# An attention and adapter kernel whose whole instruction order and PSUM bank map are written out by hand, drawn up a second time

## The chip, the core and the metric

One core of a Trainium2 chip runs the kernel. The metric is device time in microseconds (us), the median of three runs. The core has TensorE (PE in the profile, with its weight loads as PEld), VectorE (DVE), ScalarE (ACT), GpSimd (POOL) and SyncE (SP). Each engine works through its own instructions strictly in order and waits on semaphores that other engines or transfers raise. PSUM, the only memory that TensorE writes, has eight banks of 128 x 512 fp32.

## The reference

Inputs q, k, v have shape (8 batch rows, 8 heads, 576 positions, 64). In heads 0 to 3 a position attends to itself and the 31 before it; in heads 4 to 7 it attends to every fourth position of the last 128. After that comes a mixture of low-rank adapters on the heads laid side by side (512 wide), with two experts of eight chosen for each token:

```python
scores = scale * np.matmul(q, k.transpose(0, 1, 3, 2))
scores = np.where(masks[None], scores, -1e9)          # masks by head, as above
attn = np.exp(scores - scores.max(-1, keepdims=True))
attn = attn / (attn.sum(-1, keepdims=True) + 1e-9)
x = heads_side_by_side(np.matmul(attn, v))            # 4608 tokens x 512
logits = x @ w_gate                                   # 8 experts
w = softmax over the two largest logits of a token
out = x + sum over those two e of w_e * (x @ A[e]) @ B[e]   # rank 16
```

## The kernel before

The eight batch rows go through the same chain, each in two groups of four heads (g = 0 plain, g = 1 dilated). An operation has a letter, then row and group: `S121` is part 1 of the scores of row 2, group 1.

- `L`, `Lk`, `Lq`, `Lw`, `Lv`: transfers of a row's q and k, or v, from HBM into one of four input buffers, issued by POOL (lines 273, 301, 305). They turn fp32 into bf16 on the way. A row that uses a buffer again waits for the scores and products of four rows before.
- `S0`, `S1` (PE): a mask product and the scores of five and of four blocks of 64 keys, 24 and 20 load-and-multiply pairs. `E0`, `E1` (ACT, line 351): exp from two PSUM banks into bf16.
- `V` (PE, 26 pairs): exp times v in three banks, the row sum in an extra column. `R`, `N` (DVE, lines 387 and 390): reciprocal and normalisation into the fp32 row buffer. `B` (POOL, line 397): bf16 copy.
- `T`, `U` (PE): transposes. `C`, `Cd`, `Cp` (ACT): copies of them to SBUF. `Z0`, `Z1` (PE): tokens times A and the gate weights. `Y` (ACT): copy out.
- `m`, `s12`, `tt`, `top` (DVE), `th` (ACT), `g2` (DVE), `gz` (POOL; DVE in row 7): the two best experts and the weighted rank-16 vector. `G` (PE) turns it, `gc` and `gn` (ACT) copy it, `D0`, `D1`, `D2` (PE) multiply it by B. `A` (DVE) adds that to the row buffer; in late rows `dy` and `dx` (ACT) copy parts of it and POOL adds them (`A53`, `A63`, `A73`: line 559).
- `O` (SP): the row goes out. `O0` to `O5` are whole rows of 1.15 MB, rows 6 and 7 go in two halves each. Every output waits for six of the eight transfers of row 7 (`late`), and an output of a whole row waits for the last but one before it.

At the start there are constants (`con`, `cc`, `cd`: masks; `awf`, `btf`: weights; `awc`, `btc`: bf16 copies), zeroed buffers (`pz`, `vz`, `xz`, `wz`) and scratch products on a zeroed buffer that nobody reads: `warm` (five) and `F0`, `F1`, `F2`, `F3` (two, two, one, one). A scratch product is fp32 and shows as two passes in the trace.

The order is a text, `PLAN`. Its words in sequence are the order of issue on each engine, and `@n` is the first PSUM bank of an operation; an operation waits until all users of its banks' former contents have finished:

```python
for b in range(o.bank.at, o.bank.at + o.bank.size):
    o.deps = o.deps + held[b]
    held[b] = list(o.bank.users)
```

Of the kernel before, what the change touches and what calls it, by code (L numbers as in the profile page):

```python
# [37 lines left out]
ASIDE = (4, 5, 6, 7)  # L38


FILL = (("S000", 2), ("V01", 2), ("S111", 1), ("S130", 1))

# [122 lines left out]
def program(nc=None, qkv=None, aw=None, bt=None, con=None, out=None):  # L167
# [4 lines left out]
    def sb(name, shape, dt):  # L172
        return nc.alloc_sbuf_tensor(name, shape, dt) if nc is not None else None
# [16 lines left out]
    G2 = [sb(f"g2{i}", [128, 5, 8], FP) for i in range(2)]  # L190
# [29 lines left out]
    def scratch(name, n, after, each):  # L220
        k = Bank(1)
        w = WARM[:, 0:256].bitcast(FP) if nc is not None else None
        add(name, "PE", ("x", each * n, 2 * n, "f", "f"), lambda: [
            mm(bank(k), w, w[:, 0:1].to_broadcast([128, 512]), True, True) for _ in range(n)][:0], after, k)

    scratch("warm", 5, ["wz"], 1.05)
    for i, (_, n) in enumerate(FILL):
        scratch(f"F{i}", n, ["warm"], 0.86)


# [369 lines left out]


PLAN = """
pz0 wz warm@4 F1@1 awf btf vz00 pz2 con vz10 Lk00 Lk01 Lv00 Lv01
S000@6 vz01 vz11 tab cc1 cd3 vz20 cc0 vz21 cd2 cd0 L11 pz1 E000
F2@1 L10 cd1 S100@4 S101@6 E100 E101 L2 Lw2 S001@2 E001 V00@4 R00 N00 V01@1
L3 Lw3 R01 F0@0 xz0 B00 N01 B01 T00@4 vz30 L4 Lw4 pz3 C00 S111@5 E111
awc S011@2 U0@0 T01@7 E011 V11@3 Cd0 Cp0 S010@1 C01 R11 vz31 E010 N11
Z00@0 Y00 m00 Z10@6 Y10 m10 S110@4 B11 s120 E110 tt0 th0 top0 V10@2
g20 gz0 T11@5 R10 N10 btc G0@1 gc0 D01@6 B10 gn0 D00@0 C11 xz1
U1@4 Cd1 Cp1 T10@5 C10 A01 A00 S121@6 E121 S120@3 S021@1 Z01@0 E021 Z11@5  # L610
Y01 m01 Y11 m11 L5 Lw5 s121 S020@1 D02@0 V21@5 E120 top1 tt1 th1 g21
E020 A02 V20@0 R21 N21 R20 gz1 G1@5 gn1 F3@6 S130@6 N20 gc1 B21 E130
S031@3 D12@2 E031 S030@0 D10@5 T21@7 E030 C21 A12 S131@3 B20 V30@0 A10 E131
U2@7 T20@6 R30 N30 Cp2 B30 L6 Lw6 V31@3 Cd2 C20 Z02@7 Y02 Z12@1 R31
N31 B31 T30@2 D11@6 Y12 C30 S041@4 A11 E041 S141@2 S140@6 m02 E141 S040@0
m12 s122 tt2 U3@5 Cp3 th2 E040 top2 Cd3 g22 gz2 V41@2 T31@0 E140
C31 V40@5 R41 N41 Z03@2 G2@0 Y03 gn2 Z13@1 gc2 R40 Y13 N40 B40
S051@2 D20@4 E051 A20 m13 S151@6 E151 Lq700 S050@0 S150@2 E150 m03 s123 V51@5
top3 tt3 T40@3 th3 Lq701 E050 C40 B41 g23 T41@4 C41 R51 Lq710 V50@0
N51 R50 D22@5 N50 U4@7 gz3 Cd4 Cp4 G3@6 gn3 D21@3 gc3 A22 A21  # L620
Z04@7 Y04 B50 Lq711 S060@0 D32@2 Z14@7 S161@5 m04 E060 Y14 m14 E161 s124
S160@0 A32 Lv710 T50@7 E160 D30@3 S061@5 top4 V60@0 A30 tt4 R60 C50 Lv711
O1 E061 B51 T51@3 N60 C51 V61@4 th4 g24 R61 N61 U5@7 S171@2 Cp5
Cd5 S070@0 Z05@7 E171 E070 Z15@6 Y05 S170@2 S071@4 Y15 Lv700 m05 m15 top5
Lv701 B60 gz4 E170 E071 s125 G4@0 B61 D31@6 tt5 th5 gn4 V70@1 T60@4
A31 gc4 V71@5 U6@0 C60 O0 g25 O2 gz5 G5@4 Cp6 Cd6 R70 N70
B70 T61@2 D41@0 D42@3 R71 N71 gn5 A41 C61 dx4 gc5 B71 Bx7 D40@5
Z06@2 Y06 Z16@4 Y16 A40 m06 A42 D52@3 m16 s126 dx5 top6 U7@7 Cp7
Cd7 tt6 T71@1 Cx7 C71 T70@4 D51@5 A52 th6 g26 A51 D50@0 A50 C70
gz6 Z07@2 Z17 m07 m17 s127 tt7 dy5 G6@5 gc6 O3 D61@0 th7 gn6  # L630
D62@7 A53 top7 O4 dx6 g27 D60@5 gy7 gz7 A62 dy6 O5 A61 A63
O61 G7@3 H7 gm7 gn7 gc7 D72@0 dx7 A72 D71@1 A60 D73@6 O60 A71
D70@7 O71 A70 dy7 A73 O70
"""

_INS = ["qkv", "aw", "bt", "con"]
# [64 lines left out]
```

## Time and profile before

| | |
|---|---|
| median of three runs (100.13, 100.55, 100.56) | 100.55 us |
| span of the profiled execution, first to last instruction | 99.2 us |
| runs above that span | 0.9 to 1.4 us |
| PE busy, load-and-multiply pairs | 81.6 us (82%), 1587 |
| ACT busy | 71.0 us (72%) |
| DVE busy | 62.3 us (63%) |
| POOL busy | 54.6 us (55%) |
| moved by transfers | 24.5 MB |

The profiled execution is one more execution than the three; what lies around its span shows only as the difference to the runs. A busy share is a mean over a stretch in which loads arrive, a middle in which PE is nearly always busy, and an end in which outputs leave.

### The profile page before, as it was taken

To read this page: it belongs to the slowest core of one execution; us is meant where nothing else is said; L and a number is where in the kernel's file an instruction comes from. 1 tells how busy PE (TensorE), PEld (TensorE's weight loads), DVE (VectorE), ACT (ScalarE), POOL (GpSimd) and SP (SyncE) were. 2 spreads that over 40 slices of the span, in tenths; PEclk is the share of its full clock that TensorE was granted. 3 is DMA by queue.
4 is the path that set the end of the run, shared out by engine and by line. 5 is a ranking of instruction groups with operands and counts; after the bars stand their busy time and mean duration, and the time that the engine had idled before them with its cause. 6 is when DMAs were issued, how large, how long until landed. Compare 5 with 4: busy or idle time off the path is not lost.

```text
span 99.2 us, 3611 instructions
## 1 busy us (share of the span) xinstructions
PE 81.6 (82%) x1587; PEld 59.9 (60%) x1587; DVE 62.3 (63%) x138; ACT 71.0 (72%) x123; POOL 54.6 (55%) x73
## 2 busy tenths in 40 slices
PE   3999969959569989999897979999799989766200
PEld 2443457548356765779676859878687878545100
DVE  5770007706468189359746697779676999979700
ACT  5195494399938983896997679989689899757200
POOL 5999900880549136404942297099085574637800
PEclk9999999999999999999999999999999999999975
DMA  2999999999999999999999999999979988979991
GB/s 33 300 204 208 207 214 226 201 217 220 211 211 211 214 219 213 219 216 206 210 217 212 224 212 214 210 204 175 198 264 412 415 353 360 426 297 401 420 422 76
DMA packets 5807, 24.50 MB, mean 247 GB/s; under 512 B 800, under 2 KB 928, under 8 KB 5024
## 3 DMA queue, kind: packets, MB, share of 16 engines
q0 software_dynamic: 3920, 14.23, 71.9%
q1 hardware_dynamic: 1728, 9.77, 23.9%
q10 hardware_dynamic: 144, 0.28, 1.0%
q8 instruction: 12, 0.20, 0.7%
q14 instruction: 3, 0.02, 0.1%
HBM read 29.07 MB, written 9.44 MB: 388 GB/s over the span
## 4 chain that ended last, share of the span: by engine, by line
PE 57%; ACT 18%; DVE 9%; DMA 5%; issue 3%; POOL 2%; POOLq 0%
PE ps L213 49%; ACT p L351 11%; PE ps L414 5%; DMA out_dram<-x 5%; DVE x L551 4%; DVE x L390 3%; ACT xt L424 2%; PE ps L504 1%; ACT zs L472 1%; POOL x L559 1%; ACT in L263 1%; POOL xb L397 1%; PE ps L438 1%; ACT xt L427 1%; DVE top L492 1%
## 5 line engine op out<-in xcount | busy, mean ns | idle before, releaser
L397 POOL CAST xb<-x 128x1152 bf16<-128x1152 f32 (+1 forms) x16 | 18.3, 1144 | 25.4 <-DVE x L390 25.4
L351 ACT ACTIVATE p<-ps 128x960 bf16<-128x960 f32 (+1 forms) x32 | 27.6, 899 | 4.2 <-PE ps L213 4.1
L213 PE MATMUL ps<-in,p 128*64 128x130 bf16 (+1 forms) x416 | 21.5, 221 | 3.7 <-ACT p L351 3.1
L390 DVE TENSOR_TENSOR x<-ps,rec 128x1152 f32<-128x1152 f32 x16 | 21.7, 1358 | 0.5
L213 PEld LDWEIGHTS ps<-in,p 128*64 128x64 bf16 (+1 forms) x416 | 17.1, 104 | 7.2 <-ACT p L351 4.1
L551 DVE TENSOR_TENSOR x<-x,ps 128x1024 f32<-128x1024 f32 (+1 forms) x16 | 17.5, 1116 | 3.4 <-PE ps L213 3.4
L387 DVE RECIPROCAL rec<-ps 128x18 f32<-128x18 f32 x16 | 4.3, 270 | 17.5 <-PE ps L213 17.3
L213 PE MATMUL ps<-warm 128*128 128x512 f32 x22 | 13.1, 737 | 1.5 <-DVE warm L217 1.5
L499 POOL TENSOR_TENSOR gz<-zs,g 128x640 bf16<-128x640 f32 x7 | 8.9, 1275 | 9.4 <-DVE g L494 9.4
L213 PEld LDWEIGHTS ps<-in 64*64 64x64 bf16 x576 | 10.9, 106 | 2.9 <-issue 0.9
L213 PE MATMUL ps<-in 64*64 64x96 bf16 (+1 forms) x576 | 11.9, 201 | 0.7 <-issue 0.7
L273 POOL DMA_DIRECT2D in<-in_qkv_dram x22 | 11.8, 581 | 0.8 <-POOLq L684 0.8
L213 PE MATMUL ps<-aw,xt 128*128 128x136 bf16 x160 | 11.2, 223 | 0.1
L424 ACT COPY xt<-ps 128x1024 bf16<-128x1024 bf16 x8 | 8.1, 1011 | 3.4 <-PE ps L414 3.3
L213 PEld LDWEIGHTS ps<-aw,xt 128*128 128x128 bf16 x160 | 9.6, 98 | 0.9 <-ACT xt L424 0.4
L414 PE MATMUL ps<-one,xb 128*128 128x128 bf16 x128 | 9.6, 219 | 0.6 <-issue 0.5
L414 PEld LDWEIGHTS ps<-one,xb 128*128 128x128 bf16 x128 | 7.6, 97 | 2.0 <-POOL xb L397 0.7
L213 PEld LDWEIGHTS ps<-warm 128*128 128x128 f32 x22 | 4.8, 235 | 6.6 <-issue 5.0
L427 ACT COPY xt<-ps 128x1024 bf16<-128x1024 bf16 x7 | 7.2, 1033 | 1.5 <-PE ps L414 1.5
L213 PE MATMUL ps<-bt,gn 128*128 128x256 bf16 (+1 forms) x48 | 6.8, 263 | 1.6 <-ACT gn L523 0.8
L213 PE MATMUL ps<-bt,gc 128*128 128x256 bf16 (+1 forms) x48 | 6.6, 255 | 1.5 <-ACT gc L520 1.5
L472 ACT COPY zs<-ps 128x408 f32<-128x408 f32 (+1 forms) x14 | 5.9, 457 | 2.0 <-PE ps L213 2.0
(55 smaller groups left out, 101.8 us busy)
## 6 DMA issues: line engine op xcount, KB each, us to landing
out_dram<-x SPq DMA_DIRECT2D x6, 1152.0 KB, 6.1
in<-in_qkv_dram POOLq DMA_DIRECT2D x5, 1152.0 KB, 22.1
in<-in_qkv_dram POOLq DMA_DIRECT2D x10, 292.5 KB, 23.1
in<-in_qkv_dram POOLq DMA_DIRECT2D x10, 288.0 KB, 8.2
out_dram<-x SPq DMA_DIRECT2D x4, 576.0 KB, 3.8
in<-in_qkv_dram POOLq DMA_DIRECT2D x10, 146.2 KB, 8.1
in<-in_qkv_dram POOLq DMA_DIRECT2D x2, 434.2 KB, 13.7
awf<-in_aw_dram ACTq DMA_DIRECT2D x1, 272.0 KB, 3.8
```

Source lines behind the costliest of these rows:

```text
L213: return nc.tensor.matmul(o, lhsT=lhsT, rhs=rhs, start=start, stop=stop, skip_group_check=True)
L273: nc.gpsimd.dma_start(out=IN[r % SLOTS][half(a), at : at + n], in_=qkv[r, a, :, at - 2 * VB * a : at - 2 * VB * a + n],)
L351: return [nc.scalar.activation(p[:, :, :].rearrange("p h (s c) -> p h s c", c=PER)[:, :, b0 : b0 + nb, 0:SEG], PS[:, k.at : k.at + 2, 0 : ...
L387: rc = add(f"R{tag}", "DVE", ("el", 60), lambda: [nc.vector.reciprocal(rec[:, :].rearrange("p (b i) -> p b i", b=3), PS[:, k.at : k.at + 3 ...
L390: nm = add(f"N{tag}", "DVE", ("el", XG), lambda: [nc.vector.tensor_tensor(X[r][:, XG * g : XG * g + XG].rearrange("p (b i n) -> p b i n", ...
L397: add(f"B{tag}", "POOL", ("el", cut), lambda: [nc.gpsimd.tensor_copy(XB[r % 2][:, g, 0:cut], X[r][:, XG * g : XG * g + cut])], [nm] + free)
L414: nc.tensor.transpose(tp[j][:, 128 * u : 128 * u + 128], xb[:, g, 256 * u + 128 * j : 256 * u + 128 * j + 128], ident())
L424: return [nc.scalar.copy(xt[:, 0:2, 0:S].rearrange("p j (c i) -> p j c i", c=C)[:, :, :, 0:128], tp.rearrange("p j (i c) -> p j c i", c=C))]
L427: return [nc.scalar.copy(xt[:, 2:4, 0:512], tp)]
L472: zc.append(add(f"Y{st}{r}", "ACT", ("el", len(us) * ZW), lambda us=us, k=k: [nc.scalar.copy(zs[:, us[0] : us[-1] + 1].rearrange("p u n -> ...
L499: return [en.tensor_tensor(GZ[i][:, us[0] : us[0] + n, :].rearrange("p u (e r) -> p u e r", e=E), zv()[:, us[0] : us[0] + n, 0:ER].rearran ...
L551: return [nc.vector.tensor_tensor(v, v, PS[:, k.at : k.at + nk].rearrange("p b n -> p (b n)"), ALU.add)]
```

## The change

The order text is replaced. The operations stay the same but for the scratch products: `F3` is gone, and the sizes are now 2, 1, 1 for `F0`, `F1`, `F2`. In front of the first scores stand only the five products of `warm`; `F1` (one) follows `S100`, `F0` (two) stays between `V01` and `T00`, `F2` (one) goes in front of `T01`, and nothing is left in front of `S130`, where `F3` was. Each engine's own order is new, and so are most bank numbers.

```diff
@@ -38,7 +38,7 @@
 ASIDE = (4, 5, 6, 7)
 
 
-FILL = (("S000", 2), ("V01", 2), ("S111", 1), ("S130", 1))
+FILL = (2, 1, 1)
 
 
 
@@ -224,7 +224,7 @@
             mm(bank(k), w, w[:, 0:1].to_broadcast([128, 512]), True, True) for _ in range(n)][:0], after, k)
 
     scratch("warm", 5, ["wz"], 1.05)
-    for i, (_, n) in enumerate(FILL):
+    for i, n in enumerate(FILL):
         scratch(f"F{i}", n, ["warm"], 0.86)
 
 
@@ -600,37 +600,35 @@
 
 
 PLAN = """
-pz0 wz warm@4 F1@1 awf btf vz00 pz2 con vz10 Lk00 Lk01 Lv00 Lv01
-S000@6 vz01 vz11 tab cc1 cd3 vz20 cc0 vz21 cd2 cd0 L11 pz1 E000
-F2@1 L10 cd1 S100@4 S101@6 E100 E101 L2 Lw2 S001@2 E001 V00@4 R00 N00 V01@1
-L3 Lw3 R01 F0@0 xz0 B00 N01 B01 T00@4 vz30 L4 Lw4 pz3 C00 S111@5 E111
-awc S011@2 U0@0 T01@7 E011 V11@3 Cd0 Cp0 S010@1 C01 R11 vz31 E010 N11
-Z00@0 Y00 m00 Z10@6 Y10 m10 S110@4 B11 s120 E110 tt0 th0 top0 V10@2
-g20 gz0 T11@5 R10 N10 btc G0@1 gc0 D01@6 B10 gn0 D00@0 C11 xz1
-U1@4 Cd1 Cp1 T10@5 C10 A01 A00 S121@6 E121 S120@3 S021@1 Z01@0 E021 Z11@5
-Y01 m01 Y11 m11 L5 Lw5 s121 S020@1 D02@0 V21@5 E120 top1 tt1 th1 g21
-E020 A02 V20@0 R21 N21 R20 gz1 G1@5 gn1 F3@6 S130@6 N20 gc1 B21 E130
-S031@3 D12@2 E031 S030@0 D10@5 T21@7 E030 C21 A12 S131@3 B20 V30@0 A10 E131
-U2@7 T20@6 R30 N30 Cp2 B30 L6 Lw6 V31@3 Cd2 C20 Z02@7 Y02 Z12@1 R31
-N31 B31 T30@2 D11@6 Y12 C30 S041@4 A11 E041 S141@2 S140@6 m02 E141 S040@0
-m12 s122 tt2 U3@5 Cp3 th2 E040 top2 Cd3 g22 gz2 V41@2 T31@0 E140
-C31 V40@5 R41 N41 Z03@2 G2@0 Y03 gn2 Z13@1 gc2 R40 Y13 N40 B40
-S051@2 D20@4 E051 A20 m13 S151@6 E151 Lq700 S050@0 S150@2 E150 m03 s123 V51@5
-top3 tt3 T40@3 th3 Lq701 E050 C40 B41 g23 T41@4 C41 R51 Lq710 V50@0
-N51 R50 D22@5 N50 U4@7 gz3 Cd4 Cp4 G3@6 gn3 D21@3 gc3 A22 A21
-Z04@7 Y04 B50 Lq711 S060@0 D32@2 Z14@7 S161@5 m04 E060 Y14 m14 E161 s124
-S160@0 A32 Lv710 T50@7 E160 D30@3 S061@5 top4 V60@0 A30 tt4 R60 C50 Lv711
-O1 E061 B51 T51@3 N60 C51 V61@4 th4 g24 R61 N61 U5@7 S171@2 Cp5
-Cd5 S070@0 Z05@7 E171 E070 Z15@6 Y05 S170@2 S071@4 Y15 Lv700 m05 m15 top5
-Lv701 B60 gz4 E170 E071 s125 G4@0 B61 D31@6 tt5 th5 gn4 V70@1 T60@4
-A31 gc4 V71@5 U6@0 C60 O0 g25 O2 gz5 G5@4 Cp6 Cd6 R70 N70
-B70 T61@2 D41@0 D42@3 R71 N71 gn5 A41 C61 dx4 gc5 B71 Bx7 D40@5
-Z06@2 Y06 Z16@4 Y16 A40 m06 A42 D52@3 m16 s126 dx5 top6 U7@7 Cp7
-Cd7 tt6 T71@1 Cx7 C71 T70@4 D51@5 A52 th6 g26 A51 D50@0 A50 C70
-gz6 Z07@2 Z17 m07 m17 s127 tt7 dy5 G6@5 gc6 O3 D61@0 th7 gn6
-D62@7 A53 top7 O4 dx6 g27 D60@5 gy7 gz7 A62 dy6 O5 A61 A63
-O61 G7@3 H7 gm7 gn7 gc7 D72@0 dx7 A72 D71@1 A60 D73@6 O60 A71
-D70@7 O71 A70 dy7 A73 O70
+con Lk00 Lk01 Lv00 Lv01 wz tab L11 awf L10 pz3 awc cc1 warm@6 vz31 cd1
+S000@0 vz20 L2 pz0 cd2 vz01 xz0 E000 S100@3 cc0 E100 F1@6 Lw2 vz10 cd0
+cd3 S101@3 pz1 xz1 E101 S001@5 vz00 V00@0 E001 R00 N00 B00 btf vz30
+V01@5 pz2 L3 R01 N01 B01 F0@3 T00@0 C00 S111@2 Lw3 S011@4 E011 E111 L4
+F2@1 T01@7 C01 Lw4 U0@6 Cp0 Cd0 vz11 V11@0 R11 N11 Z10@6 Y10 m10 btc
+Z00@7 Y00 S110@4 m00 s120 E110 B11 tt0 S010@0 top0 L5 E010 th0 g20 T11@3
+V10@4 R10 N10 vz21 gz0 C11 G0@0 gc0 B10 gn0 S121@1 E121 D02@6 A02 D00@3
+A00 U1@2 T10@0 Cp1 Cd1 C10 S021@5 D01@1 Lw5 E021 Z01@0 A01 Y01 Z11@7 Y11
+S020@1 m11 m01 top1 s121 tt1 th1 g21 gz1 E020 S120@3 E120 V21@5 S030@0
+E030 V20@2 R21 L6 N21 G1@5 gn1 S130@0 E130 B21 R20 N20 Lw6 D10@6 A10
+S031@1 gc1 E031 S131@3 D12@0 E131 A12 B20 U2@7 Cd2 T20@5 C20 Cp2 V30@0
+T21@3 C21 R30 N30 B30 V31@4 Lq711 Z12@7 R31 N31 B31 Y12 m12 Lq710 S141@0
+E141 D11@2 A11 T30@7 C30 Z02@6 Y02 m02 S041@4 E041 s122 tt2 th2 top2 g22
+S040@0 E040 Lq701 S140@6 E140 V41@2 T31@1 R41 N41 U3@0 Cp3 Cd3 V40@5 R40
+N40 gz2 G2@0 C31 Z03@1 Lv710 Lq700 gn2 B41 gc2 Y03 Z13@4 Y13 m03 m13
+top3 s123 B40 S151@2 S051@0 D20@5 E151 Lv711 E051 A20 O1 S050@2 E050
+T41@7 S150@0 V51@4 Lv700 U4@3 tt3 th3 C41 g23 gz3 R51 N51 E150 T40@7 C40
+V50@0 R50 N50 G3@7 Cd4 Cp4 Z14@6 gc3 Y14 Lv701 Z04@3 m14 gn3 Y04 m04
+S060@5 E060 D22@2 A22 B51 T51@1 C51 D21@3 A21 B50 U5@0 S161@6 O0 Cp5 Cd5
+top4 E161 s124 T50@5 S160@1 D30@3 C50 D32@0 E160 A32 S061@6 E061 Z15@5
+A30 tt4 th4 V60@0 R60 Y15 S171@6 N60 V61@3 R61 m15 N61 E171 S071@6 E071
+O2 Z05@2 Y05 g24 m05 B60 S070@0 B61 s125 tt5 gz4 S170@4 E070 D31@6 E170
+A31 th5 T61@3 C61 V70@0 U6@7 R70 Cp6 Cd6 top5 T60@3 g25 G4@4 N70 V71@5
+R71 C60 N71 Z06@3 gc4 gn4 Y06 Z16@1 Y16 m06 m16 s126 D42@0 top6 dx4 tt6
+D41@2 A41 Bx7 O3 gz5 G5@6 gc5 B70 T70@4 U7@5 th6 D40@0 Cp7 gn5 Cd7 g26
+C70 A42 A40 O4 B71 D50@2 dy5 A50 T71@6 Cx7 D51@0 A51 gz6 G6@4 A53 C71
+D52@2 gn6 dx5 A52 Z07@5 m07 Z17 m17 D60@2 O5 gc6 D62@1 dy6 s127 tt7 th7
+top7 g27 gz7 dx6 gy7 G7@0 H7 gn7 A63 gm7 A62 A60 O60 D61@6 D73@2 gc7
+D71@4 A61 O61 D72@1 A71 D70@0 dx7 A72 dy7 A70 A73 O71 O70
 """
 
 _INS = ["qkv", "aw", "bt", "con"]
```

## Rows read from the trace of the kernel before

**Rows 1.** Page: GB/s that the transfers moved, in 40 slices of 2.48 us.

```profile
GB/s 33 300 204 208 207 214 226 201 217 220 211 211 211 214 219 213 219 216 206 210 217 212 224 212 214 210 204 175 198 264 412 415 353 360 426 297 401 420 422 76
```

**Rows 2.** Page: DMA queue of instructions; packets, MB, share of 16 engines' span.

```profile
q8 instruction: 12, 0.20, 0.7%
```

**Rows 3.** Busy time by stretch: PE, PEld, DVE, ACT, POOL; PEclk, DMA share, GB/s.

```profile
23.00:45.00 22.00, 19.06 (x446) 14.62 (x445) 13.86 (x33) 17.82 (x30) 9.04 (x10) 1.00 1.06 215
45.00:70.20 25.20, 23.06 (x552) 18.56 (x547) 18.69 (x43) 21.01 (x34) 15.24 (x19) 1.00 1.04 208
```

**Rows 4.** Timeline of PEld, first 13 us: start, duration, instruction, [idle before].

```profile
1.49 0.50 PEld L213 LDWEIGHTS ps<-warm 128*128 128x128 f32 x2 [1.49 <-DVE warm L217]
...
6.78 0.21 PEld L213 LDWEIGHTS ps<-warm 128*128 128x128 f32 x1 [0.52 <-issue]
7.22 0.19 PEld L213 LDWEIGHTS ps<-warm 128*128 128x128 f32 x1 [0.24 <-issue]
...
10.33 0.11 PEld L213 LDWEIGHTS ps<-one 64*64 64x64 bf16 x4 [0.76 <-issue]
```

**Rows 5.** DMA issues begun at 1.92 and at 7.01: KB, us to landing.

```profile
in<-in_qkv_dram POOLq DMA_DIRECT2D x1, 288.0 KB, 6.0
...
in<-in_qkv_dram POOLq DMA_DIRECT2D x1, 146.2 KB, 11.4
```

**Rows 6.** Timeline of PE, 16 to 40 us.

```profile
16.59 1.94 PE L213 MATMUL ps<-warm 128*128 128x512 f32 x4
...
18.99 0.36 PE L213 MATMUL ps<-con,one 64*64 64x384 bf16 x4
...
26.56 1.33 PE L213 MATMUL ps<-in,p 128*64 128x130 bf16 x26 [1.21 <-ACT p L351]
...
38.61 1.08 PE L213 MATMUL ps<-warm 128*128 128x512 f32 x2
```

**Rows 7.** Timeline of ACT, 22.9 to 25 us.

```profile
22.96 1.16 ACT L263 COPY in<-warm 64x1170 f32<-64x1170 f32 x1
24.15 0.97 ACT L351 ACTIVATE p<-ps 128x960 bf16<-128x960 f32 x1
```

**Rows 8.** Timeline of PEld, 47 to 71 us.

```profile
47.15 0.45 PEld L414 LDWEIGHTS ps<-one,xb 128*128 128x128 bf16 x8
...
52.78 0.37 PEld L414 LDWEIGHTS ps<-one,xb 128*128 128x128 bf16 x6 [0.63 <-issue]
...
58.74 0.11 PEld L213 LDWEIGHTS ps<-in 64*64 64x64 bf16 x3 [0.87 <-issue]
...
70.18 0.15 PEld L213 LDWEIGHTS ps<-in,p 128*128 128x128 bf16 x2 [0.67 <-issue]
```

**Rows 9.** DMA queue of instructions in the window 50.3 to 51.4 us.

```profile
q8 instruction: 1, 0.02, 5.4%
```

**Rows 10.** Timeline of all engines, 75.8 to 99.2 us.

```profile
77.98 1.34 PE L213 MATMUL ps<-in,p 128*64 128x130 bf16 x26
...
85.97 1.36 PE L213 MATMUL ps<-aw,xt 128*128 128x136 bf16 x20
...
86.56 1.27 POOL L559 TENSOR_TENSOR x<-x,in 128x512 f32<-128x512 f32 x1
...
88.18 0.24 ACT L491 ACTIVATE th<-tt 128x40 f32<-128x40 f32 x1
...
92.98 1.26 POOL L559 TENSOR_TENSOR x<-x,btf 128x512 f32<-128x512 f32 x1 [0.24 <-DMA out_dram<-x]
```

**Rows 11.** DMA issues running at 88.0 and at 94.4: KB, us to landing.

```profile
out_dram<-x SPq DMA_DIRECT2D x1, 1152.0 KB, 5.0
...
out_dram<-x SPq DMA_DIRECT2D x1, 576.0 KB, 4.1
```

**Rows 12.** Busy time by stretch (columns as in rows 3), end of loads, outputs.

```profile
71.50:73.50 2.00, 1.98 (x63) 1.61 (x60) 1.97 (x4) 1.58 (x5) 1.22 (x2) 1.00 0.60 153
...
90.00:97.50 7.50, 1.68 (x20) 1.09 (x17) 3.48 (x5) 2.09 (x5) 3.81 (x4) 0.87 0.96 395
```

## The prediction

> **What bounds the kernel now.** I read the page first. The bandwidth by slice shows two regimes [rows 1]: loads at about 213 GB/s from 5 us to 72 us without a hole, then outputs at about 400. So the transfers are busy all the time, and a gain in the arithmetic can only come out where an engine is late behind them. Next the table by stretch [rows 3]. From 23 to 45 us PE is busy 19.06 of 22.00 us and ACT 17.82; from 45 to 70.2 PE is busy 23.06 of 25.20. Up to 23 us the chain runs after landings; from 23 to 45 PE and ACT pass waits to each other; from 45 on PE alone sets the pace until the last exp-times-v product, V71, which ends at 79.32 (77.98 + 1.34) [rows 10]. After it comes a chain of some 15 us through DVE, ACT, PE and POOL to the last output.
>
> The third view is PE's own idle time. Three holes in the busy stretch have no releaser, only "issue": before 52.78, 58.74 and 70.18 [rows 8]. Each lies inside one operation (six of T31's eight transposes, three of S050's 24 pairs and two of V60's 26 are still to come), so no semaphore explains it. Counting pairs in the old order, they are at pairs 856, 982 and 1236: 126 and twice 127 apart. The instruction queue moved 12 packets in all [rows 2], 1587 pairs over 12 packets are 132 a packet, and one packet moved between 50.3 and 51.4, shortly before the first hole [rows 9]. I read these holes as PE out of instructions until the next packet is in. Pair 728 was at 47.2 (two transposes into T30) [rows 8], so the stretches between packet edges took 5.6 us (728 to 856), 6.0 (856 to 982) and 11.4 (982 to 1236). If a packet cannot be turned around in less than about 5.7 us, PE's pace in the dense stretch is set by that and by no order.
>
> **The change part by part.** All sums are differences to the profiled span of 99.2 us; they are then taken from the median of 100.55, which lies 1.3 above it.
>
> *Front.* Two products, four passes of 0.43 us (6.78 to 7.22) [rows 4], go. Of the ten left, six start at the slow pace before 6.78 and four run after it, so S000 can begin at 6.78 + 4 x 0.435 = 8.5 in place of 10.33. Its own q and k land at 1.92 + 6.0 = 7.9 [rows 5], so the landing allows it: -1.8 us. That gain meets the next landing. The last piece of L11 lands at 7.01 + 11.4 = 18.4 [rows 5]; S111 began at 18.99, queued behind F0 (1.94 us) and T00 [rows 6]. In the new order F0 starts some 1.6 us earlier and T00 is over by 17.5, so S111 starts at the landing: -0.6, the whole of what the front can hand on. What else moved there is hidden: awf goes behind the table load, so awc, now in front of pz0, vz01, vz10, pz1 and vz00 on DVE, ends near 6.8, and these end near 11, before V00 at about 12.3. Should awf be 1.3 us later still, V00 slips with it, and the 0.6 stays untouched until T00 is 0.9 late.
>
> *Rows 0 to 3.* A zeroing copy of 1.16 us on ACT (vz31) stood in front of E010 [rows 7]; it moves into the idle front, and vz21 comes in behind th0, where ACT would wait for T11 and gz0 anyway: 0. F2, about 1.0 us now in front of T01, is covered by the exps that V11 waits for; without that cover it would cost up to 1.0. Walking the new order with durations of the trace: S111 18.4, S011 to 19.4, E011 (0.97) [rows 7] and E111 to 21.2, V11 (1.33) to 22.55, Z10 and Z00 (1.36) to 23.95, S110 and S010 to 24.9, E110 and E010 to 26.2. So V10 begins at 26.25 where it began at 26.56 [rows 6]: -0.3. Half the gain has gone, because Z now stands in front of the scores and E010 is the last exp instead of E110. On the way to V20 the new order puts more in front of it (D01, S120, S030, and th1 ahead of E020, so E020 waits for the chain m, s12, tt): V20 is about 0.3 late. Then F3 is missing (1.08 us) [rows 6], and V30 and V31 come out 0.6 to 0.7 early. In front of V31 both orders hold the same set of operations but for the scratch products. After V31 the new order brings only Z12 and 18 pairs of S141 to pair 728: 46.2 to 46.5 in place of 47.2. I take -0.85; the bounds are -1.0 (no wait for a packet) and 0 (the 0.3 waits before V10 and V20 doubled).
>
> *Rows 4 to 7.* Without packet holes the same walk brings pair 1236 (in V60) at 68.2, -2.0. With the packet interval the gain stays what it was at pair 728, because the old order was at the packets' pace from 728 to 1236 (23.0 us for 508 pairs) and the new one needs the same packets: -0.85. The Trainium skill bears on this, "Runtime: NRT & Kernel Launch", section "Instruction fetch mechanics": blocks of 16 KiB are fetched while the block before runs, and crossing an edge is "mostly hidden". By that rule the sum at pair 1236 would be -2.0; the trace disagrees in three places with 0.5 to 0.7 us of PE idle each [rows 8]. I go by the rows. From pair 1236 to the end of V71 the new order has 221 pairs, the old 207 (T61 and U6 now stand ahead of V70 and V71): +0.45 at some 31 pairs a microsecond. V71 ends at -0.4.
>
> *The end.* Counted from V71's end, the old order had Z07 at 6.65, th7 at 8.86, A53 over at 8.51 and A73 over at 14.92 [rows 10]. Walked with the same durations the new one has Z07 at 6.5, th7 at 8.95 (behind gc6 and dy6 on ACT), A53 over at 7.2 with A52 at 8.2, A73 over at 15.05. The last outputs keep the transfers full, 0.96 from 90 to 97.5 [rows 12]; O5, which starts that train and took 5.0 us to land [rows 11], leaves 0.3 earlier, the last one leaves 0.1 later and took 4.1. I take -0.25, bounds -0.5 and +1.2 (below).
>
> *Loads and outputs.* POOL issues row 7's loads behind V31 and not between casts near the end. Slices 26 to 28 ran at 204, 175 and 198 GB/s [rows 1]; against 213 that is (9 + 38 + 15) / 213 x 2.48 = 0.7 us, which the first output may win. It does not reach the end, since O5 waits for A53: 0, bound -0.7. The pause between loads and outputs (share 0.60 in 71.5 to 73.5) [rows 12] stays, as the same six transfers hold back O1.
>
> Sum: -0.85 + 0.45 - 0.25 = -0.65, so 100.55 - 0.65 = 99.9.
>
> **The rivals.** *The packets don't bind.* If the holes were put there by something else, or fall where PE waits anyway, the -2.0 at pair 1236 stands, with +0.45 - 0.25 a total of -1.8; transfers left unused 0.8 us at 71.5 to 73.5 [rows 12], and the earlier loads give 0.7, so they allow about 1.5 to 1.8: 98.8. Against it: three holes, evenly spaced in pairs. It is what the section of the Trainium skill named above ("Runtime: NRT & Kernel Launch", "Instruction fetch mechanics") leads one to expect. *Nothing arrives.* The 0.6 from L11's landing is used up by V20 (the walk has it 0.3 late there already), F3's 1.08 us only lay where PE waited for exps, and the packets keep the old pace: 0, 100.5. For it: ACT is at 81% from 23 to 45 [rows 3], and every exp has a copy in front. *Slower: ACT in the tail.* The new ACT order puts dy5 before C71, and gn6, dx5, gc6, dy6 before th7. If gn5, which D50 and so dy5 wait for, ends more than about 0.4 us later than in my walk, C71 and Z07 slip by 0.85 and th7 waits for dy6 another 0.5; G7, H7 and all that follow on the last chain move 1.2 to 1.4 us. Less the 0.4 at V71 that gives 101.3. For it: five more copies stand in one engine's queue ahead of a step that everything left waits for. Against: in the walk D50 is over 0.3 to 0.4 us before ACT gets to dy5, a small margin, but it is there.
>
> **How the numbers follow.** Likeliest 0.46 at 99.9, its own range 99.4 to 100.4. Packets not binding 0.16 at 98.8. Nothing 0.20 at 100.5. Slower 0.18 at 101.3. A half per cent, 0.5 us, is about what can be told from no change: faster means under 100.05, slower over 101.05. Of the likeliest, two thirds lie below 100.05: 0.30; with 0.16 that is 0.46, rounded 0.47. The rest of the likeliest, 0.16, and most of nothing, 0.17, give 0.32; slower 0.18 and the upper edge of nothing, 0.03, give 0.21. The range 98.7 to 101.3 holds the likeliest, nothing, most of the first rival and half of the slower one.
>
> **What would show it.** S000 at 8.2 to 8.6; S111 at 18.3 to 18.5, whatever came before; V10 near 26.2, V20 near 37.2, V31 near 44.0; PE idle with "issue" alone inside U3 or V40, T41 and V60 (pairs 856, 982, 1236), at 51.5 to 52.5, 57.5 to 58.5 and 69 to 70; V71 over near 78.9; th7 near 88; the last output issued near 94. If the holes sit at other pairs or are gone, the packet step is wrong and the time is below 99.4. If V31 is not before 44.4, the middle gave nothing. If th7 is more than 9.5 us behind V71's end, the tail has become the bound. A PE clock below 1.00 in the stretches before 90 us, where every row shown has 1.00 [rows 3, 12], would mean that the missing products were needed after all: then every PE term here is wrong, and upwards.

## The result and the profile after

| | before | after |
|---|---|---|
| median of the runs | 100.56 us (4 runs) | 104.40 us (103.61 to 104.83, 4 runs) |
| ratio, 95% interval | | 1.038 (1.032 to 1.044) |
| span of the profiled execution | 99.2 us | 102.7 us |
| V71 over | 79.32 | 81.82 |
| last output leaves, lands | 94.32, 98.43 | 98.96, 101.87 |

The kernel is 3.8% slower; 99.9 was forecast, with 101.3 as the upper end. Times here and below are medians of all runs; disturbed executions are left out of every ratio, and the traces of e2, e3, c3 and q2 show such ones. In the two traces the loss has two places: 2.50 us at V71's end and another 0.94 from there to the last landing, 3.44 together.

The page first: GB/s by slice, the granted clock by slice, the instruction queue.

```profile
PEclk9999999999999999999999999999999999998555
GB/s 44 273 208 206 210 221 205 215 213 215 212 216 210 218 212 213 216 212 216 218 208 216 215 213 215 210 208 183 196 438 416 409 384 32 280 401 269 397 296 201
q8 instruction: 12, 0.20, 0.7%
```

Loads run at the same 213 GB/s to the same time [rows 1]; the output phase has a new gap (32 GB/s in slice 33). Busy time by stretch, columns as in [rows 3]:

```profile
23.00:45.00 22.00, 18.58 (x448) 14.42 (x446) 14.40 (x33) 18.48 (x30) 10.64 (x12) 1.00 1.06 215
45.00:70.20 25.20, 22.02 (x516) 17.83 (x520) 16.09 (x41) 20.09 (x36) 13.39 (x16) 1.00 1.05 213
...
86.00:88.00 2.00, 1.49 (x16) 1.26 (x17) 2.00 (x4) 2.00 (x5) 1.54 (x2) 1.00 0.00 0
...
94.00:96.00 2.00, 1.64 (x11) 0.75 (x8) 1.50 (x2) 0.54 (x2) 0.00 (x0) 0.56 0.65 270
```

Up to 45 us as many pairs are done as before; from 45 to 70.2 PE does 516 in place of 552 and is busy a microsecond less. The clock is 1.00 until 94 us, when it falls to the lower level. From the timeline of PEld, where S000 begins:

```profile
7.94 0.11 PEld L213 LDWEIGHTS ps<-one 64*64 64x64 bf16 x4 [0.90 <-DMA in<-in_qkv_dram]
```

From the timeline of PE, S111, V10 and the end of V71 (80.48 + 1.34 = 81.82):

```profile
18.62 0.36 PE L213 MATMUL ps<-con,one 64*64 64x384 bf16 x4 [1.38 <-DMA in<-in_qkv_dram]
...
26.32 0.77 PE L213 MATMUL ps<-in,p 128*64 128x130 bf16 x18
...
80.48 1.34 PE L213 MATMUL ps<-in,p 128*64 128x130 bf16 x26
```

S000 begins 2.4 us earlier [rows 4], at the landing of its q and k; S111 waits for its landing and begins 0.37 earlier, V10 0.24 [rows 6]. Next the holes, from the timeline of PEld, 45 to 73 us:

```profile
45.99 0.36 PEld L213 LDWEIGHTS ps<-in 64*64 64x64 bf16 x15
46.92 0.10 PEld L213 LDWEIGHTS ps<-in 64*64 64x64 bf16 x1 [0.57 <-issue]
...
53.18 0.10 PEld L414 LDWEIGHTS ps<-one,xb 128*128 128x128 bf16 x1 [1.10 <-issue]
...
59.41 0.37 PEld L414 LDWEIGHTS ps<-one,xb 128*128 128x128 bf16 x6 [0.93 <-issue]
...
66.07 0.19 PEld L213 LDWEIGHTS ps<-in 64*64 64x64 bf16 x12 [0.75 <-issue]
...
71.86 0.87 PEld L213 LDWEIGHTS ps<-in,p 128*64 128x64 bf16 x17 [0.36 <-issue]
```

Where the old kernel has three holes without a releaser [rows 8], this one has five, in S141, T31, T41, S060 and V60. Counted in pairs they are at 729, 855, 983, 1108 and 1235. Measured between the starts of neighbouring weight loads beyond the usual 0.05, they are 0.63, 1.15, 0.97, 0.80 and 0.42, in sum 3.97 us (before: 0.68, 0.93 and 0.72, 2.33).

The chain of waits, from V71's end to the last output (start, duration, what):

```profile
84.07 0.50 DVE top L492
84.57 0.55 DVE tt L489
85.13 1.13 DVE x L551
86.26 0.11 DVE g L494
86.37 1.14 DVE x L551
87.51 0.05 issue
87.56 0.61 PE ps L213 x4
...
90.92 0.25 ACT th L491
91.17 0.02 issue
91.20 1.24 DVE g L494
...
93.07 0.75 PE ps L504 x10
...
94.60 1.86 PE ps L213 x9
...
97.62 1.26 POOL x L559
```

A41 and A40 (L551) now stand behind row 6's selection (`top6`, `tt6`) on DVE, so A40 is over at 87.5 and O4 leaves at 87.53 (before 83.92); hence the two microseconds at 0 GB/s. `g27`, 0.20 us before, takes 1.23. The timeline of all engines shows what runs beside it, and how long four products took at the lower clock, 1.06 us in place of 0.60 to 0.61 elsewhere:

```profile
91.11 1.26 POOL L559 TENSOR_TENSOR x<-x,in 128x512 f32<-128x512 f32 x1 [0.90 <-ACT in L557]
91.20 1.23 DVE L494 SCALAR_TENSOR_TENSOR g<-th,top 128x40 f32<-128x40 f32 x1 [0.33 <-ACT th L491]
...
95.00 1.06 PE L213 MATMUL ps<-bt,gc 128*128 128x256 bf16 x4
```

### The profile page after: what moved, and what is told of

It is laid out like the page before. It is cut to its first block, busy times and chain, and to the rows that moved or that the text cites. A ratio compares the mean times of both kernels' runs of the same rounds, so it can differ in the third digit from the quotient of the medians.

```text
span 102.7 us, 3601 instructions
## 1 busy us (share of the span) xinstructions
PE 81.2 (79%) x1583; PEld 59.7 (58%) x1583; DVE 63.1 (61%) x138; ACT 71.2 (69%) x123; POOL 54.0 (53%) x73
## 4 chain that ended last, share of the span: by engine, by line
PE 35%; DMA 28%; DVE 11%; ACT 11%; POOL 5%; issue 5%; POOLq 0%
PE ps L213 29%; DMA in<-in_qkv_dram 28%; ACT p L351 6%; DVE x L390 4%; PE ps L414 3%; POOL in L273 3%; DVE x L551 2%; PE ps L504 2%; ACT xt L424 2%; DVE g L494 1%; POOL x L559 1%; POOL xb L397 1%; ACT xt L427 1%; DVE rec L387 1%; ACT zs L472 1%
## 5 line engine op out<-in xcount | busy, mean ns | idle before, releaser
L397 POOL CAST xb<-x 128x1152 bf16<-128x1152 f32 (+1 forms) x16 | 17.8, 1114 | 27.1 <-DVE x L390 27.0
L551 DVE TENSOR_TENSOR x<-x,ps 128x1024 f32<-128x1024 f32 (+1 forms) x16 | 17.7, 1116 | 2.3 <-PE ps L213 2.1
L414 PE MATMUL ps<-one,xb 128*128 128x128 bf16 x128 | 10.1, 219 | 2.5 <-issue 1.7
L213 PE MATMUL ps<-warm 128*128 128x512 f32 x18 | 10.9, 741 | 1.2 <-DVE warm L217 1.2
L213 PE MATMUL ps<-bt,gn 128*128 128x256 bf16 (+1 forms) x48 | 7.3, 278 | 2.8 <-ACT gn L523 1.5
L213 PE MATMUL ps<-con,one 64*64 64x384 bf16 (+1 forms) x64 | 6.0, 362 | 2.8 <-DMA in<-in_qkv_dram 1.4
L523 ACT COPY gn<-ps 128x576 bf16<-128x576 bf16 (+2 forms) x9 | 5.2, 593 | 3.4 <-PE ps L504 3.4
L472 ACT COPY zs<-ps 128x272 f32<-128x272 f32 (+1 forms) x14 | 6.2, 455 | 1.7 <-PE ps L213 1.6
```

The costliest lines, as they stand in the source:

```text
L213: return nc.tensor.matmul(o, lhsT=lhsT, rhs=rhs, start=start, stop=stop, skip_group_check=True)
L397: add(f"B{tag}", "POOL", ("el", cut), lambda: [nc.gpsimd.tensor_copy(XB[r % 2][:, g, 0:cut], X[r][:, XG * g : XG * g + cut])], [nm] + free)
L414: nc.tensor.transpose(tp[j][:, 128 * u : 128 * u + 128], xb[:, g, 256 * u + 128 * j : 256 * u + 128 * j + 128], ident())
L472: zc.append(add(f"Y{st}{r}", "ACT", ("el", len(us) * ZW), lambda us=us, k=k: [nc.scalar.copy(zs[:, us[0] : us[-1] + 1].rearrange("p u n -> ...
L551: return [nc.vector.tensor_tensor(v, v, PS[:, k.at : k.at + nk].rearrange("p b n -> p (b n)"), ALU.add)]
```

## The experiments

Theory A (A1 beside A2 below) from these rows: PE cannot get its next packet of instructions sooner than some 6 us after the last one while loads run, whatever the order; an order that reaches the edge of a packet early is starved there, and again at each edge after it. Rivals: row 7's loads, now queued earlier on POOL, slow the packets or the loads (A2); the missing scratch products cost something; the new end alone makes the loss.

**Row 7's loads put back late, and the same loads put early in the old order.**

```diff
 e1_late7 (new order)
-... V31@4 Lq711 ... m12 Lq710 ... E040 Lq701 ... Lv710 Lq700 ... Lv711 ... Lv700 ... Lv701
+... B40 Lq711 Lq710 ... gz3 Lq701 ... B50 Lv710 Lq700 Lv711 Lv700 Lv701
 e2_early7 (old order)
+... gz2 Lq711 Lq710 Lq701 Lv710 Lq700 Lv711 ... B40 Lv700 Lv701
```

> The new order with one thing put back: POOL issues row 7's eight transfers behind B40, gz3 and B50 (about 58 to 69 us) in place of behind B30 to gz3 (46.7 to 61.8); PE, ACT and DVE orders stay as in the new kernel. Theory A2 (the instruction packets take longer because row 7's loads are queued so early): the holes without a releaser at T31, T41, S060 and V60 shrink from 1.1, 1.0, 0.8 and 0.5 us to the 0.5 to 0.7 of the kernel before, V71 ends at 80.0 to 80.5 in place of 81.8, and the time is 102.6 to 103.0. Theory A1 (the packets are slow beside any loads, whenever these were issued): holes unchanged within 0.2 us, V71 at 81.5 to 82.0, time 104.1 to 104.7.

> The cross test: the old order, with row 7's eight transfers issued early, behind gz2 and B40 (about 52.7 to 58.5 us in place of 57.4 to 69.3). A2: the holes in S050, S060 and V60 grow by 0.3 to 0.5 us each, V71 ends about 1.0 to 1.5 later than 79.3 and the time is 101.5 to 102. A1: V71 stays at 79.3 within 0.3; the loads are in up to 0.7 us earlier, and the time is 100.2 to 100.7.

Measured: e1 103.91 us, ratio to before 1.026 (1.014 to 1.037, overlapping with the changed kernel's), holes of 1.52, 1.14, 0.98 and 0.79 at the first four edges, V71 over at 82.31. e2 100.92, ratio 1.003 (0.997 to 1.008). The place of these loads is not the cause; A2 falls. A1 holds at three of the four holes; the first grew by 0.9, and V71 and the time lie 0.3 and 0.2 outside its ranges. e1's trace shows one thing more: from 67 to 69 us, where its transfers are busy only 0.60 to 0.67 of the time, the packet after the edge at 67.01 starts 1.7 us behind that edge, in place of 3.8 to 4.3 behind the three before it, and the next edge has no hole.

**No loads beside the middle.** Loads of rows 4 to 7 left out in both orders; the outputs wait for S171.

```diff
     def loads(r):
+        if r >= SLOTS:
+            for g in range(2):
+                qk_ready[r, g], v_ready[r, g] = [], []
+            return
...
+    late.append("S171")
```

> The new order without the loads of rows 4 to 7: these rows compute on the data that rows 0 to 3 left in the buffers, and the outputs, which had waited for row 7's loads, wait for S171. Theory A (PE runs out of instructions because its packets queue behind loads): from about 40 us, when row 3 is in, to S171 no hole without a releaser is over 0.2 us; a packet follows its edge by under 2.5 us in place of 3.5 to 4.3; V71 ends 3.5 to 4.5 us earlier than 81.8. Theory B (the new order's own waits between PE, ACT and DVE set the pace): V71 at 81 or later, with the idle time moved to waits that have a releaser.

> The kernel before without the loads of rows 4 to 7 (they compute on what rows 0 to 3 left; outputs wait for S171), the partner of the run of the new order without them, in which V71 ended at 77.97. Theory A: no holes without a releaser; the old order loses its 1.8 to 2.3 us of holes less what other waits take up, so V71 at 77.4 to 78.4, at most 0.5 away from the new order's. Then without packets the two orders are alike and the packets make all of the 2.5. Theory D (the new middle is slower in itself): V71 at 76.5 or below.

Measured, one run each: new order 101.12, old order 100.06. Busy time from 45 to 68 us, the new order (e5):

```profile
45.00:68.00 23.00, 22.47 (x543) 18.52 (x544) 17.17 (x42) 21.17 (x37) 9.45 (x8) 1.00 0.01 3
```

The same for the old order (e9):

```profile
45.00:68.00 23.00, 22.09 (x536) 17.85 (x537) 16.85 (x43) 19.93 (x34) 9.31 (x8) 1.00 0.01 3
```

With the transfers idle (share 0.01) no hole of over 0.2 us without a releaser is left in either at the packets' edges, though the pairs and packets are the same. In e5 a packet starts 0.3 to 1.5 us behind its edge, in the changed kernel 3.5 to 4.3 while loads run. PE is past the edge near pair 1236 at 67.9 us in the new order, where the walk without packets had 68.2, and at 68.1 in the old: up to there the two orders are alike without loads, and the holes come of packets that have to get through beside loads. V71 is over at 77.97 in the new order and 77.22 in the old. These 0.75 us, more than the 0.5 that Theory A allowed, arise behind pair 1236, where the new order has T61 and U6 in front of V71. The Trainium skill ("Runtime: NRT & Kernel Launch", "Instruction fetch mechanics") has them "mostly hidden": true of these two runs, not of the kernels with loads.

**The edges moved.** 40 one-column scratch pairs behind F1 shift every later operation against the packets.

```diff
+    for h in range(2):
+        kp = Bank(1)
+        add(f"X{h}", "PE", ("x", 1, 20, "f", "f"), lambda h=h, kp=kp: [
+            mm(PS[half(i % 2), kp.at, i : i + 1], WARM[half(h), 0:64], WARM[half(h), 0:1], True, True) for i in range(20)][:0], ["wz"], kp)
...
-... E100 F1@6 ...
+... E100 F1@6 X0@7 X1@2 ...
```

> The new order with 40 scratch pairs of one column more, behind F1, where PE waits 1.2 us for S101 anyway. A (holes at the edges of instruction packets): they stay at the same pair counted from the start (about 729, 855, 983, 1108, 1235) and so move 40 pairs back in the order: out of S141, T31, T41, S060 and V60 into V31 or Z12, V41, D20 or S050, Z14 or Z04, and D30 to S061. If something about those operations makes the holes, they stay in S141, T31, T41, S060 and V60, at pairs 769, 895, 1023, 1148 and 1275. The time stays within 0.7 us of 104.4 in both.

Measured, one run: 105.92 us, above the 0.7 around 104.4 that was expected. Three of the holes, timeline of PEld:

```profile
50.69 0.14 PEld L213 LDWEIGHTS ps<-in 64*64 64x64 bf16 x6 [0.81 <-issue]
...
57.28 0.18 PEld L213 LDWEIGHTS ps<-in 64*64 64x64 bf16 x10 [0.90 <-issue]
...
63.34 0.10 PEld L213 LDWEIGHTS ps<-in,p 128*128 128x128 bf16 x1 [0.67 <-issue]
```

They stand at pairs 856, 983 and 1110, within two of the changed kernel's, but in S140, S051 and V50; a fourth (1.72) is at 1236, in S061. At 729 there is none here. The holes belong to the count of instructions and not to an operation or its banks.

**The orders spliced.** New up to V31 and then old (c1), new up to V71 and then old (c3), old up to T61 and then new (c2).

```diff
 c1_newfront: words of the new order to V31@4, then the old order's other words
 c3_new_oldtail: words of the new order to V71@5, then the old order's other words
 c2_old_newtail: words of the old order to T61@2, then the new order's other words
```

> The new order and banks up to V31, from there the old ones for all that is left (scratch products as in the new kernel). It has the front's gain (V31 ends 0.5 earlier than in the kernel before, 45.5 in place of 46.0) and the old middle and end. Theory A (from the edge at pair 728 on the packets of instructions set the pace, so an early arrival there is worth nothing): V71 ends at 79.0 to 79.8 against 79.3, time 100.2 to 100.9. Rival D (the new middle order itself costs the 2.5 us, and the front's gain is real): V71 at 78.6 to 78.9, time 99.8 to 100.1.

> The new order up to V71, the old one behind it (A41 and A40 ahead of m06 to tt6 and g2 of row 6; dy5 behind C70, th7 ahead of dy6; A53 and A63 where they were). If the new end costs 0.95 us by itself (19.1 us from V71's end to the last output's landing before, 20.05 after), V71 ends at 81.5 to 82.4 and the last landing follows by 18.9 to 19.3: time 103.2 to 103.8. If the end is as long whatever its order because the outputs bound it, it follows by 19.8 to 20.2: 104.1 to 104.8.

> The cross test: the old order up to T61, the new one behind it (G5 where the new one has it). If the new end costs 0.95 us by itself: V71 at 79.3, time 101.2 to 101.8. If it costs nothing in a kernel whose V71 is early: 100.3 to 100.8.

Measured: c1 101.59, ratio 1.008 (1.005 to 1.011); c3 103.05, 1.020 (1.013 to 1.027); c2 104.36, 1.035 (1.029 to 1.042). c1's holes (PEld):

```profile
47.56 0.10 PEld L414 LDWEIGHTS ps<-one,xb 128*128 128x128 bf16 x1 [0.26 <-issue]
...
53.52 0.15 PEld L414 LDWEIGHTS ps<-one,xb 128*128 128x128 bf16 x2 [1.09 <-issue]
...
60.02 0.11 PEld L213 LDWEIGHTS ps<-one 64*64 64x64 bf16 x3 [1.24 <-issue]
```

V31 is over at 45.66 there, 0.36 early, and V71 at 80.95, 1.6 late, with everything behind V31 in the old kernel's order: 1.0 late by pair 1236, the rest with a wait of 0.93 for a DVE normalisation before 75.63 that the old kernel has not. So the new front by itself turns its gain into a loss, a small one (0.8%). The new end taken off the new kernel gives back about 1.8%. c2's 3.5% is no price of the new end: its chain goes from V71 through T61, a copy and Z06 to row 6's selection, while the changed kernel has T61 ahead of V70; th7 begins 11.03 us behind V71's end (9.10 in the changed kernel), and the last landing follows by 21.97 (20.05). All three forecasts of the time missed, c3's by 0.15.

**The scratch products alone.** Taken out of the old order (p1), put back into the new one (p2).

```diff
 p1_old_noscratch (old order)
-pz0 wz warm@4 F1@1 awf ... S000@6
+pz0 wz warm@4 awf ... S000@6
 p2_new_scratch (new order)
-... warm@6 vz31 cd1 S000@0
+... warm@6 vz31 cd1 F3@1 S000@0        (F3: two products)
```

> The old order and old banks, with the two scratch products in front of S000 taken out and nothing else changed: the headline of the change alone. Theory A (PE is starved at every instruction packet once it reaches an edge early): S000 starts near 8.5 instead of 10.33, S111 at L11's landing (18.4 to 18.6), the middle is 0.3 to 0.6 us early at pair 728 (T30), a hole of 0.3 to 0.6 us appears there, and what follows is not earlier than in the old kernel or up to 0.8 us later, as in the kernel that had the new order up to V31 (0.8 % slower): 100.5 to 101.3 us. Rival B (what costs is the new order of operations, not the earlier arrival): the 0.4 to 0.6 us of the front stay and the kernel takes 100.0 to 100.2 us. A third possibility: the products were needed for the clock; then the clock in the records falls below 1.00 before 20 us.

> The new order with two scratch products put back in front of S000, nothing else changed. S000 starts near 9.7 instead of 7.95 and S111 is 0.3 to 1.0 us later. Theory A (packets set the pace, the time is fixed from the first starved edge on): V31 ends 0.3 to 0.8 us later than in the changed kernel, the hole in S141 is smaller by about as much, and from the hole in T31 on both run alike: V71 within 0.4 us of 81.8, the time 104.0 to 104.8. Rival B (the earlier front is itself what costs, because PE loses its lead at pair 728): without the hole in S141 the later edges come 0.5 us or more earlier each, V71 ends near 80.5 to 81.2 and the time is 103.0 to 103.7.

Measured: p1 100.67 beside 100.78, ratio 0.998 (0.995 to 1.002). p2 103.86, ratio 1.026 (1.020 to 1.033). PEld of p1 at its holes:

```profile
58.09 0.11 PEld L213 LDWEIGHTS ps<-one 64*64 64x64 bf16 x3 [0.71 <-issue]
...
70.01 0.39 PEld L414 LDWEIGHTS ps<-one,xb 128*128 128x128 bf16 x7 [0.94 <-issue]
```

V71 in p1's timeline of PE:

```profile
77.60 1.34 PE L213 MATMUL ps<-in,p 128*64 128x130 bf16 x26
```

PEld of p2 at the first edge:

```profile
47.70 0.13 PEld L213 LDWEIGHTS ps<-in 64*64 64x64 bf16 x5 [0.89 <-issue]
```

In p1 V31 is 0.5 us early, pair 728 is crossed at 46.9 without a hole, and V71 is 0.38 early [rows 10]: in this one trace the gain lasts, as the prediction had it, though over twelve runs it can't be told from none. The 0.5 at V31 is no larger than the scatter: other traces of the old front have it over at 45.54 (e2) to 46.38 (c2). The hole that Theory A put at 728 did not appear; neither did Rival B's time. In p2 the hole in S141 is larger (0.95), which neither expected, V71 is over at 82.01, which is Theory A's number, and the time lies between the two forecasts. Put back, the scratch products change the ratio from 1.038 to 1.026, with intervals that just touch; taken out of the old order they cost nothing. The order makes the loss.

**Inside the new end.** A62 in front of A63 on POOL (e3); A40's add cut to 64 columns (q2).

```diff
 e3_tail
-... gn7 A63 gm7 A62 A60 ...
+... gn7 gm7 A62 A63 A60 ...
 q2_a40cut
+                if (r, g) == (4, 0):
+                    return [nc.vector.tensor_tensor(v[:, 0:64], v[:, 0:64], PS[:, k.at, 0:64], ALU.add)]
```

> The new order with one exchange on POOL: A62 in front of A63. In the new kernel g2 of row 7 took 1.22 us in place of 0.20, beginning 0.09 us behind A63's start (91.11) and ending 0.05 us behind its end (92.37). Theory C (that DVE instruction, with two inputs in SBUF, is held while POOL works): A62 can't begin before dx6 ends (91.43), so g27 begins alone and takes 0.20 us; gz7, G7 and the rest move 1.0 us forward and the time is 103.2 to 103.6. Rival (POOL's A63, A62 and then O60 bound the end, or the outputs do): g27 is short but the end stays, 104.2 to 104.6.

> The new order with the add A40 cut from 1024 columns to 64 (so the output of row 4 is not complete in its other columns); it is the add that holds row 4's output and D51 back until 87.5 us in the changed kernel. Theory E (the chain A41, A40, D51, G6 behind row 6's selection on DVE sets the end): O4 leaves near 86.4 instead of 87.53, D51, G6 and the copies behind it come 0.6 to 1.1 us earlier, th7 and G7 too, and the time is 103.3 to 103.8. Rival (the end is set by Z07's branch and by g27, which stands beside A63 on GpSimd): O4 leaves 1.1 us earlier, but G7 and the last output move by 0.3 us or less, and the time is 104.0 to 104.6.

e3's `g27` and A63 (timeline of all engines):

```profile
91.78 0.20 DVE L494 SCALAR_TENSOR_TENSOR g<-th,top 128x40 f32<-128x40 f32 x1 [0.33 <-ACT th L491]
...
92.77 1.27 POOL L559 TENSOR_TENSOR x<-x,in 128x512 f32<-128x512 f32 x1
```

With POOL out of its way `g27` is back at 0.20. G7 follows V71's end by 10.2 us in place of 11.25, and the last output leaves at 97.75, 15.3 behind V71 in place of 17.1; but it takes 4.6 us to land, 19.94 behind V71 in all (20.05), and e3's times (103.47 to 105.10) scatter too widely to price it. So the hold is real; e8 below shows what it is worth in the total. In q2 O4 leaves 4.70 us behind V71's end in place of 5.71, while `g27` still takes 1.23 and G7 comes 11.03 behind V71 (11.25): the rival's reading. The time, 104.85 with a ratio of 1.029 (1.022 to 1.036), overlaps with the changed kernel's, so no gain is claimed for it. From these two traces only distances within each are used.

**Fewer pairs.** Masks by two 128 x 128 products in place of four 64 x 64, in the new order (e6), the old one (e7), and with A62 first (e8).

```diff
-                for pr, a, c in tiles:
-                    mm(PS[half(c), k.at + pr, 0 : nb * SEG], ident(a), mask(a), True, False)
+                for pr in range(2):
+                    mm(PS[:, k.at + pr, 0 : nb * SEG], ident(), mask(), True, False)
```

> The same edit in the new order. A: 32 pairs fewer ahead of the first starved edge (S141) and 24 fewer from there to V60: V71 ends 1.2 to 1.8 earlier than 81.8, time 102.5 to 103.2. B: V71 within 0.3 of 81.8, time 104.0 to 104.8.

> The old order with fewer PE instructions for the same work: each score operation adds its mask with two products of 128x128 (both halves of the partitions at once, the mask is the same in both) in place of four of 64x64, so it has 22 and 18 pairs in place of 24 and 20; 64 pairs of 1587 go, the columns that stream through PE in that time stay about the same (0.36 to 0.40 us an operation before). Theory A (in the dense stretch a block of some 127 pairs takes about 6.2 us, since the next packet of instructions is not there earlier): fewer pairs are worth time though PE works no less; the holes in T31, S050 and V60 shrink or go, V71 ends 0.8 to 1.2 earlier than 79.3, time 99.4 to 99.9. Theory B (the work of the array sets the pace): V71 within 0.3 of 79.3, time 100.3 to 100.9.

> The new order with the two-product masks and with A62 in front of A63 on POOL. If g27's 1.2 us beside A63 lie on the chain that ends last, this is 0.8 to 1.1 us below the run with the masks alone; if the outputs bound the end, it is the same within 0.4.

Measured: e6 106.33, ratio 1.052 (1.046 to 1.058); e7 107.63, 1.066 (1.061 to 1.072); e8 105.98, 1.049 (1.043 to 1.055). e6 and e7 are slower than their parents, and both forecasts missed. e8 lies 0.35 us below e6, within the 0.4 that was expected if the outputs bound the end: `g27` takes 0.20 in e8 and 1.23 in e6, G7 comes 1.0 earlier behind V71, and the last landing follows V71's end by 20.08 and 20.03. What slows e6 and e7 is in each score operation (e7, PEld):

```profile
40.79 0.23 PEld L213 LDWEIGHTS ps<-in 64*64 64x64 bf16 x16 [0.32 <-issue]
41.07 0.11 PEld L213 LDWEIGHTS ps<-con,one 128*128 128x128 bf16 x2
41.58 0.27 PEld L213 LDWEIGHTS ps<-in 64*64 64x64 bf16 x20 [0.40 <-issue]
```

At the change from products on the whole array to 64 x 64 tiles the next weight load stands 0.32 or 0.40 us, 32 times in the kernel, 11.4 us in sum; PE meanwhile finishes the mask products. That outweighs 64 pairs fewer, and says nothing on Theory A.

## Why the prediction was wrong

*Front*: the gain was there, by another path than forecast. S000 began at 7.94 and not at 8.2 to 8.6: the scratch passes reached the faster pace at 5.56 and not at 6.78, the last began at 6.86, and the landing of q and k ended the wait, not the products. S111 stood at L11's landing as forecast, 18.62 (18.3 to 18.5).

*Rows 0 to 3*: right in PE's arrival. V10 26.32 (26.2), V20 37.48 (37.2), V31 44.21 (44.0), and PE stood in front of pair 729 at 46.24, as forecast (46.2 to 46.5). It then waited until 46.92, where the old order crossed at 47.15: of the -0.85 only some -0.2 was left. These are single traces: V31 was over at 45.54 to 46.38 in four of the old front and at 45.54 to 46.52 in seven of the new, so the front's gain is no larger than that scatter.

*Rows 4 to 7* is the step that failed: "With the packet interval the gain stays what it was at pair 728". Two things were wrong in it. First, it counted the interval from pair 728, where the old order was not starved. The edge before, pair 601, is crossed at 41.0 us by both orders, counted in the two traces. The new order runs the 127 pairs after it in 5.3 us, the old one in 6.2. The packet started at 44.5 in both and would let PE go on at about 46.9, 5.9 us behind the edge. The gain at 728 was made inside one packet interval and could not be kept. Second, the interval was taken as 5.7. In the new trace PE goes on after the edges at 46.92, 53.18, 59.41, 66.07 and 71.86: 5.9, 6.3, 6.2, 6.7 and 5.8 us, a mean of 6.18 from 41.0, starved at each. The old order, starved at three of five, took 29.2 us over the same five, 5.84 each [rows 8]. Five times 0.34 is 1.7 us: PE is past the edge near pair 1236 at 71.86 and not 70.18, +1.7 where the prediction had -0.85. The holes at 855, 983 and 1235 were forecast, those at 729 and 1108 were not. Other traces agree: the same five intervals take 29.5 and 29.7 us in p1 and c2 (old order up to there), 30.1 in c1, and 30.5 and 31.2 in p2 and e1 (new order). Without loads the two orders stand within 0.2 us of each other at this edge (e5, e9), so the 1.7 is made by packets beside loads.

Why the new order's intervals are longer is seen only in part. At every hole of over 0.3 us PE goes on 2.2 to 2.5 us after a packet's start. The start itself varies: at the edges up to pair 1108, e1's pause apart, it comes 3.5 to 4.4 us behind a starved edge (5.1 once, in e4) and 2.5 to 4.4 behind one that PE crosses without a hole. From hole to hole it takes 5.8 to 6.7 us (7.5 once, in e4), from an edge without a hole to the next hole 5.2 to 6.8. The old order has its short intervals there, 5.6 and some 5.3 us behind the edges at 728 and near 1109 [rows 8]; the new one, starved at every edge, gets none. That is a tendency and no rule: from the edge at 601, which no order starves at, it takes 6.5 us in c1 and 6.8 in e1. Why the request comes later is not shown. p1 is the counterpart of the change: as early at V31 (over at 45.52, 45.55 in the changed kernel), slower behind pair 601 (6.4 us), no hole at 728, no loss.

The +0.45 for T61 and U6 in front of V71 was mis-sized: from pair 1236 to V71's end the new order takes 9.96 us, the old 9.14, so +0.8 (and 0.9 without loads, e5 beside e9). Counted in the traces 221 and 215 pairs lie there, not 221 and 207, and the old order does them at 23.5 a microsecond, not 31; PE also waits 0.44 us for `B60` before 77.60, which the walk did not have. V71 is over at +2.5, not -0.4.

*The end* failed too: from V71's end to the last landing 20.05 us against 19.11, +0.94 where -0.25 was forecast. To the departure of the last output it is even +2.1 (17.14 against 15.00); three parts make it up. `g27` beside A63 costs 1.0, shown by e3. The lower clock from 94 us on costs about 0.8: p2, the same order but for two scratch products, kept 1.00 there, its four products of D71 took 0.60 in place of 1.06, and its last output left 16.37 behind V71 (timeline of PE):

```profile
95.00 0.60 PE L213 MATMUL ps<-bt,gc 128*128 128x256 bf16 x4
```

Some 0.3 remains for the rest (th7 0.25 later). Not all of this reaches the landing, since the last output then takes 2.9 us to land in place of 4.1. There the clock's part is what shows: the last landing follows V71's end by 19.29 in p2 and e1, which kept 1.00 until PE's last products. The hold of `g27` does not show there: without it the last output leaves earlier and takes 4.6 us (e3) and 4.0 (e8) to land, 19.94 and 20.08 behind V71. The walk had durations of the old trace for every operation and looked at queues and semaphores only; it did not ask which POOL operation would run beside a DVE operation. The Trainium skill has that rule ("SBUF — State Buffer", "Terms": DVE and GpSimd share a pair of ports, held for a whole instruction, and the other waits in full); this trace agrees, 1.23 against 0.20 us. It was not weighed. That O4 leaves 3.6 us later also went unseen, as the step followed only V71's successors. In q2, where O4 leaves 1.0 us earlier behind V71, the last landing still follows by 20.12; what it costs together with the rest is not settled.

*Loads and outputs*: 0, as forecast. The last load that O1 waits for (Lv711) lands at 72.51 (72.28), slices 26 to 28 run at 208, 183 and 196 GB/s [rows 1]; the 0.7 held as possible did not come.

Of the rivals, *The packets don't bind* erred to the other side: they bind harder than the prediction took. *Slower* had the right side, but its mechanism did not happen: Z07 begins 6.79 us behind V71's end (6.65), th7 is over at 9.35 (9.10). Of the chance for a slower kernel, 0.21, all but 0.03 hung on that one mechanism in the tail; a loss in the packets was given none, since the old order's interval was let stand as the worst case.

## What to carry to other kernels

When an engine is out of instructions at regular counts, list the time between edges for every stretch, starved or not: an order that packs a stretch between two edges tighter than a packet's turnaround (5.3 against 5.9 us here) gains nothing there and can lose at every later edge, as this one did. Price such a stretch by the packets, and let the order's gain fall where a packet is already in. When an order is redrawn from measured durations, go through the operations that become neighbours in time on DVE and POOL, since a duration measured alone is not kept beside the other.

## What the runs showed of the hardware

- Instruction packets beside loads: five holes of 0.4 to 1.15 us within 26 us; none with the loads of rows 4 to 7 left out, where a packet started 0.3 to 1.5 us behind its edge in place of 3.5 to 4.3.
- From a packet's start to PE's going on it took 2.2 to 2.5 us at every hole of over 0.3 us; from one hole's end to the next 5.8 to 6.7 us (7.5 once), from an edge crossed without a hole 5.2 to 6.8.
- At the change from 128 x 128 products to 64 x 64 tiles inside an operation the next weight load stood 0.32 us behind mask products of 384 columns and 0.40 behind those of 480, all 32 times.
- A DVE operation on 40 columns with two SBUF inputs took 1.23 us beside a POOL add of 1.26, and 0.20 without it.
- The granted clock fell from 1.00 to 0.50 (the lower of its two levels) at 94.25 us in the profiled execution of the new order and stayed at 1.00 until PE's last product in that of p2, with two more scratch products at the start; in both PE had stood 2.4 us in front of G7.
